# Moving weight loads, their homes and the work behind them: w2a ahead of w2b's third unit, w2b's fifth unit in the loop

## The reference

```
state = gamma*state + k_t v_t^T ;  y_t = q_t state / sqrt(D)          # x = [3072, 512]
logits = x @ phi ; d = softmax over tokens ; slot_input = d.T @ x      # 32 slots, 4 for each of 8 experts
slot_out[e] = relu(slot_input[e] @ w1a[e]) @ w2a[e]                    # w1a [8,512,1024], w2a [8,1024,512]
x2 = softmax over slots(logits) @ slot_out
noisy = x2 @ w_gate + log1p(exp(x2 @ w_noise)) * noise ; top 2 of 8
out[token] += weight * (relu(x2[token] @ w1b[e]) @ w2b[e])             # w1b [8,512,1024], w2b [8,1024,512]
```

## Time and profile before

| | |
|---|---|
| median of 3 runs | 618.42 us (618.32 to 619.48) |
| the profiled execution, its own time | 620.97 us |
| its span, first to last instruction | 619.3 us |
| PE busy | 526.3 us, 85% |
| DVE, ACT, POOL busy | 276.9, 193.1, 250.3 us |
| mean granted TensorE clock | 0.916 of full |
| DMA moved | 107.88 MB, mean 174 GB/s |

### The profile page before, as it was taken

How to read it: one execution, slowest core, us unless ns; L and a number is a source line. 1 busy time by engine, 2 the same in 40 slices (tenths; PEclk the granted TensorE clock), 3 DMA queues, 4 the chain that set the end, 5 groups by cost and what they waited for, 6 DMA issues and landing times.

```text
span 619.3 us, 13374 instructions
## 1 busy us (share of the span) xinstructions
PE 526.3 (85%) x4842; PEld 309.7 (50%) x4843; DVE 276.9 (45%) x427; ACT 193.1 (31%) x357; POOL 250.3 (40%) x218
## 2 busy tenths in 40 slices
PE   4989989796871456575999999999999999999992
PEld 4767667674451343242445545554555445455451
DVE  3536456553654056954578333333323323332330
ACT  0212112121466142464695222222222222222120
POOL 1222122121010000306556766766666666666553
PEclk9989999998795666776999999999999999999997
DMA  6889897886897999958241222212223331433410
GB/s 234 291 278 338 305 335 272 320 299 223 293 380 270 387 399 404 411 237 283 57 151 39 51 44 49 53 35 44 52 43 56 47 47 30 52 44 44 54 18 2
DMA packets 48803, 107.88 MB, mean 174 GB/s; under 512 B 11481, under 2 KB 12745, under 8 KB 48768
## 3 DMA queue, kind: packets, MB, share of 16 engines
q1 hardware_dynamic: 34512, 92.89, 41.6%
q0 software_dynamic: 14256, 14.49, 13.3%
HBM read 93.87 MB, written 29.70 MB: 200 GB/s over the span
## 4 chain that ended last, share of the span: by engine, by line
PE 72%; DMA 14%; DVE 5%; issue 3%; ACT 2%; SPq 0%; POOL 0%; DVEq 0%; ACTq 0%
PE ps L862 45%; DMA w_region<-moe_w 8%; DMA w_region<-chunks 5%; PE ps L845 4%; PE ps L618 3%; PE ps L574 3%; PE ps L721 3%; PE ps L613 3%; PE ps L604 2%; PE ps L625 2%; DVE w_region L1249 1%; PE ps L777 1%; PE ps L648 1%; DMA ident_stack<-consts 1%; PE ps L587 1%
## 5 line engine op out<-in xcount | busy, mean ns | idle before, releaser
L862 PE MATMUL ps<-w_region,s_region 128*128 x1320 | 296.6, 381 | 1.2 <-ACT s_region L1038 1.2
L862 PEld LDWEIGHTS ps<-w_region,s_region 128*128 128x128 f16 x1320 | 127.6, 98 | 146.2 <-issue 5.8
L1432 DVE SCALAR_TENSOR_TENSOR s_region<-ps,s_region 128x1024 f16<-128x1024 f32 x55 | 67.3, 1224 | 184.8 <-ACT s_region L1038 181.9
L1038 ACT ACTIVATE s_region<-ps 128x1024 f16<-128x1024 f32 x55 | 56.3, 1024 | 79.5 <-PE ps L845 50.2
L542 POOL DMA_INDIRECT out<-s_region,rec_region x42 | 71.5, 1702 | 13.5 <-issue 12.5
L536 POOL DMA_INDIRECT out<-s_region,rec_region x42 | 47.4, 1129 | 66.8 <-DVE s_region L1446 66.8
L530 POOL DMA_INDIRECT rec_region<-records,idx x55 | 58.0, 1054 | 18.5 <-issue 18.5
L1028 ACT ACTIVATE s_region<-rec_region 128x128 f16 (+1 forms) x55 | 17.0, 309 | 129.5 <-DMA rec_region<-records,idx 129.5
L744 PE MATMUL ps<-w_region,sw_region 128*32 128x128 f32 x512 | 23.2, 358 | 29.9 <-DMA w_region<-moe_w 29.3
L470 POOL TENSOR_TENSOR s_region<-w_region,s_region 128x512 f32<-128x512 f32 x14 | 14.6, 1044 | 62.5 <-DMA w_region<-chunks 58.5
L1446 DVE TENSOR_SCALAR s_region<-ps,rec_region,y_scale 128x512 f32<-128x512 f32 x42 | 33.9, 806 | 6.4 <-PE ps L862 4.0
(11 more groups left out here) (221 smaller groups left out, 605.5 us busy)
## 6 DMA issues: line engine op xcount, KB each, us to landing
w_region<-moe_w SPq DMA_DIRECT2D x19, 2048.0 KB, 17.0
w_region<-chunks SPq DMA_DIRECT2D x32, 512.0 KB, 6.6
w_region<-moe_w SPq DMA_DIRECT2D x24, 512.0 KB, 7.4
s_region<-moe_w SPq DMA_DIRECT2D x5, 2048.0 KB, 19.1
sw_region<-chunks SPq DMA_DIRECT2D x16, 512.0 KB, 6.3
s_region<-moe_w SPq DMA_DIRECT2D x4, 512.0 KB, 6.9
w_region<-moe_w SPq DMA_DIRECT2D x2, 1024.0 KB, 6.7
out<-s_region,rec_region POOLq DMA_INDIRECT x84
```

The costliest lines, as they stand in the source:

```text
L862: last = nc.tensor.matmul(bank[6 + r], h[:, r, f, :], w2b_parts[:, bass.ds(e, 1), part, f, :].rearrange("p e m -> p (e m)"), start=(first ...
L1038: nc.scalar.activation(h_hi[:, r, :, :].rearrange("p c t -> p (c t)").rearrange("p (a n) -> p a n", a=2), ps[:, 2 + 2 * r:4 + 2 * r, :], A ...
L1432: nc.vector.scalar_tensor_tensor(out=h_lo[:, r, :, :].rearrange("p c t -> p (c t)").rearrange("p (a n) -> p a n", a=2), in0=ps[:, 2 + 2 * ...
```

## The change

Parts of it, with the new line numbers:

- **Loads.** The order is w2b 0, w2b 1, w2a 0 to 7, w2b 2, w1b 0 to 3, w2b 3, w1b 4 to 7, w2b 4 to 7. Every unit has a semaphore of its own, and new homes: w2a in units 4, 5, 6, 8, 2, 3, 4, 5; w1b in 6, 3, 4, 5, 6, 4, 5, 6; w2b arrives in 9, 7, 8, 7, 5, 6, 7, 8. The load of w1b 7 waits for the product with w1b 4. The loads of w2b 6 and 7 wait for the low part of w2b 3.
- **Division.** The slots are no longer divided by their sums before the w1a products; the ReLU's output is multiplied by the inverse instead (one number for each of its rows). The sum over the four row groups is a product with a small matrix `same`, after the first w1a product.
- **PE order.** The c transposes come after the third w2a product. After sort third 0 and the spreads of experts 0 and 1 come w1b 4, sort thirds 1 and 2, the spreads of 2 and 3, w1b 5 to 7.
- **w2b.** Unit 2's sums stand behind softplus, its high half ahead of `sw_sums(0)`; unit 3's sums behind `sw_high(3)`, its high half ahead of `sw_sums(5)`; unit 3's second low half, and all of unit 4 to 7, come in the loop. Units 2 and 3 are summed in two pieces.

```diff
-        w2b_in = [stage_b, w_ring[3], stage_a, stage_b, stage_a, w_ring[2], w_ring[3], stage_a]
+        w1a_home = [unit(u) for u in (4, 5, 6, 0, 8, 1, 2, 3)]
+        w2a_home = [unit(u) for u in (4, 5, 6, 8, 2, 3, 4, 5)]
+        w1b_home = [unit(u) for u in (6, 3, 4, 5, 6, 4, 5, 6)]
+        w2b_in = [unit(u) for u in (9, 7, 8, 7, 5, 6, 7, 8)]
...
 # SyncE: load_w2b(e), load_w2a(e), load_w1b(e)
                 elif e == 2:
-                    sp.wait_ge(ring_used, DC + 1)
-                elif e <= EARLY:
-                    sp.wait_ge(w2b_lo_ready, 1 if e == 3 else 3)
-                elif e < E - 1:
-                    sp.wait_ge(ring_used, 2 * E + e + 2)
+                    sp.wait_ge(ring_used, E + 4)
+                elif e == 3:
+                    sp.wait_ge(w2b_lo_ready, 2)
+                elif e < 6:
+                    sp.wait_ge(ring_used, 2 * E + e + 3)
                 else:
-                    sp.wait_ge(w2b_lo_ready, EARLY + 1)
+                    sp.wait_ge(w2b_lo_ready, 4)
...
+            def load_w2a(e):
+                sp.wait_ge(ring_used, (1, 2, 3, 5, 7, 8, E + 1, E + 2)[e])
...
+            def load_w1b(e):
+                sp.wait_ge(ring_used, (E + 3, E + 6, E + 7, 2 * E, 2 * E + 1, 2 * E + 3, 2 * E + 4, 2 * E + 5)[e])
...
 # ScalarE
-                if e < EARLY:
-                    act.wait_ge(ring_used, DC + e + 1 if e > 0 else DC)
-                elif e < EARLY + 2:
-                    act.wait_ge(ring_used, 2 * E + e + 1)
+                if e <= EARLY:
+                    act.wait_ge(ring_used, (4, 6, E + 5, 2 * E + 2, 2 * E + 6)[e])
                 else:
                     act.wait_ge(w2b_lo_ready, e)
...
+            w2b_sums(4, junk)
             h_high(1, 1)
...
-                if i in (3, 5):
-                    w2b_sums(EARLY + (i + 1) // 2, junk)
-                if i in (4, 6, 8):
-                    w2b_high(EARLY + i // 2 - 1)
+                if i in (4, 6):
+                    w2b_sums(4 + i // 2, junk)
+                if i in (3, 5, 7, 8):
+                    w2b_high({3: 4, 5: 5, 7: 6, 8: 7}[i])
...
 # VectorE
-            join_den()
-            dve.wait_ge(den_spread, 1)
-            link(nc.vector.tensor_scalar(inv_den[:, :], bank[0][:, 0:SL], 1e-9, None, ALU.add))
-            link(nc.vector.reciprocal(inv_den[:, :], inv_den[:, :]))
             dve.wait_ge(slot_in_turned, 1)
...
-            nc.vector.tensor_scalar(h1_4, bank[5][:, 0:F // REP], 0.0, None, ALU.max).then_inc(h1_kept, 1)
+            nc.vector.tensor_scalar(h1_4, bank[5][:, 0:F // REP], 0.0, inv_den[:, 0:1], ALU.max,
+                                    ALU.mult).then_inc(h1_kept, 1)
...
+                if i == 0:
+                    w2b_low(3, (1,))
+                if i in (0, 2, 4, 5):
+                    e = {0: 4, 2: 5, 4: 6, 5: 7}[i]
                     w2b_scale_by_sum(e)
                     scale_y(slice(e, e + 1))
-                if i in (0, 2, 4, 6):
-                    w2b_low(EARLY + i // 2)
+                if i in (1, 3, 5, 6):
+                    w2b_low({1: 4, 3: 5, 5: 6, 6: 7}[i])
```

More of the change, by code:

```diff
@@ L453, in _ @@
             for e in range(E):
-                load_ring(w2a, e, E + e)
-                if e in (2, 5):
-                    load_w2b(2 + e // 5)
+                load_w2a(e)
+            load_w2b(2)
             for e in range(E):
-                load_ring(w1b, e, 2 * E + e)
+                load_w1b(e)
                 if e == 3:
-                    load_w2b(EARLY)
-            for e in range(EARLY + 1, E):
+                    load_w2b(3)
+            for e in range(EARLY, E):
                 load_w2b(e)
@@ L509, in _ @@
             nc.gpsimd.memset(h1_blocks, 0.0).then_inc(blocks_zeroed, 1)
-            for e in range(EARLY):
+            for e in range(3):
                 w2b_all_sum(e)
@@ L724, in _ @@
                 last.then_inc(ring_used, 1)
-            pe.wait_ge(c_ready, 1)
-            for i in range(NT // REP):
-                last = nc.tensor.transpose(bank[2 + i // 4][:, i % 4 * P:(i % 4 + 1) * P],
-                                           c_prob[:, i * REP:(i + 1) * REP, :].rearrange("p t s -> p (t s)"), ident[:, :])
-            last.then_inc(c_turned, 1)
+                if e == 0:
+                    pe.wait_ge(den_ready, 1)
+                    nc.tensor.matmul(bank[0][:, 0:2], same, den[:, :], start=True, stop=True).then_inc(den_spread, 1)
             pe.wait_ge(h1_kept, 1)
@@ L812, in _ @@
                              stop=True).then_inc(ranks_done, 1)
-            for e in range(1, 6):
+            for e in range(1, 4):
                 sw_product(e)
@@ L1009, in _ @@
                 sw_high(e)
+            w2b_sums(3, junk_mid)
+            for unit in range(4):
+                sw_keep(unit)
+            sw_sums(4)
+            act.wait_ge(w2b_sum_ready, w2b_sums_of(4))
+            for unit in range(4, 8):
+                sw_keep(unit)
+            w2b_high(3)
             sw_sums(5)
-            w2b_high(EARLY)
-            for unit in range(8):
-                sw_keep(unit)
             sw_sums(6)
@@ L1280, in _ @@
             w2b_low(0)
-            for e in range(1, EARLY):
-                w2b_scale_by_sum(e)
-                w2b_low(e)
+            w2b_scale_by_sum(1)
+            w2b_low(1)
             dve.wait_ge(iotas_ready, 6)
```

136 lines of the change are left out of this document (67 added, 69 removed).

## The result

The changed kernel takes 614.25 us, median of 20 runs (610.46 to 619.17), against 619.48 us (614.61 to 622.71) for the kernel before in 20 runs on the same chip: ratio 0.9922, interval [0.9897, 0.9947]. The forecast was 608.3, range 603.8 to 613.2. It is faster, as forecast, but by 5.2 us instead of 10.1, and the time lies 1.1 us above the range. The forecast started from 618.42, the median of three runs; with the ratio taken on that start the time would be 613.6, still above the range. Ratios here compare the fast runs of both kernels; a run more than 1.5% above the fastest of its kernel is left out of them.

The account below looks back on a forecast made before the run. DMA supply was taken to bound the stretch ahead of the loop, PE alone the loop. A loop start 14.5 us earlier less 4.4 us of loop stalls gave 10.1 us off 618.42: 608.3 us, range 603.8 to 613.2.

Parts of the forecast that it names:

- w2a's loads: Weight loads ahead of the ranks: w2a 7 lands 17.3 us earlier, from two w2b units (10.5), the hole (5.4), the division (1.3).
- the stretch from the ranks to the loop: From the rank product at 226.8 to the loop start at 277.0, a loop start 14.5 us earlier than before.
- the first stall: In the loop at tile 5's turn, PE waits 2.6 us because w2b 6's load lands late and holds up ACT.
- The hole of 5.4: DMA supply gap between w2a 2 and w2a 7, where SP waits for w2b's low part; removing it gains 5.4 us.
- The division: Slot reduction ahead of w1a starts at once, without the division's chain: 1.3 us gained for w1a and the loads behind.
- Up to the ranks: From the last w2a product's start to the rank product: 18.5 us of DVE, ACT and PE work, unchanged.
- ACT becomes late: Between ranks and group 0's scales, unit 2's high half queues ahead of w1b's first sums on ACT, costing 1.3 us.
- The last w1b unit and the tail: Ahead of the loop: w1b 7 lands at 264.2, group 1's scales come at 264.5, the loop starts 12.5 us later.
- Second stall: In the loop at tile 9's turn, PE waits 1.8 us because unit 6's later low part delays ACT's unit 7 half.
- Rival 2: Products before the loop run at half clock and ACT's queue is longer: 3 to 6.8 us less gain, 611.5 to 615.1; chance 0.20.
- Rivals 1, 3 and 4: No loop stalls, 603.9 (0.14); w2b 6 landing after 24 us, 622.3 (0.05); supply not holding front, no change (0.05).

Follow-up runs that it names:

- e3: Changed kernel with w2b 2 loaded right behind w2a 2 again and w2a 3 waiting in unit 7's buffer: 623.01 us, ratio 1.0052 to the kernel before.
- e1: Changed kernel with the second low half of w2b 3 done ahead of the token loop: 610.88 us, ratio 0.9875 to the kernel before.
- e2: Changed kernel with w2b 3's second low half ahead of the loop and unit 7's high and low halves one tile later: 611.64 us, ratio 0.9872.
- e5: The kernel before, unchanged, run and profiled once more: ratio 1.0008 to the kernel before.
- e4: The kernel before with only the division moved behind w1a's products, into the ReLU: 620.06 us, ratio 0.9997 to the kernel before.
- e7: Changed kernel with the high half of w2b 2 behind the first four w1b sums on ScalarE instead of ahead: 617.21 us, ratio 0.9953 to the kernel before.

## Why the prediction was right and wrong

Where it failed: three terms of the sum were mis-sized (w2a's loads, the stretch from the ranks to the loop, the first stall), and one is missing (the slow products behind that stall).

- **Mechanism and places: right.** e3 shows that the order of the loads carries the front, e1 and e2 that the loop gives back what w2b 6 and the low part of unit 6 make it wait. No gap that wasn't forecast appears in the first nine tiles; what appears is a slow product.
- **w2a's loads: mis-sized, 14.9 us instead of 17.3.** Counted from T the mean goes from 69.7 to 54.8. From w2a 2 to w2a 7 the gain was 14.5 us instead of 16.0. The hole of 5.4 came from one execution with 42.3 us from w2a 2 to w2a 7; e5 and e4 had 40.7 and 40.4. And a unit took 5.40 us (27.00 for five, from the rows above), not 5.27, so that seven of them leave 4.5 us for the hole in the first profile and 3.0 in e5. The division brought 0.4 us up to w2a 2 instead of 1.3. The kernels of the later runs that are the same up to there put it at about 0.8, and the gain at w2a 7 at 15.2.
- **Up to the ranks: 18.5 us, right on average** (19.6, 18.6, 17.0).
- **ACT becomes late: too dear by 1.4.** Group 0's scales came 16.8 behind the ranks, not 18.2; e7 shows why.
- **The last w1b unit and the tail: 1.2 us too cheap, with the 1.4 us above counted in.** Ranks to loop was forecast as 50.2 us; it was 49.6, 52.7 and 52.6, against 47.4 and 47.8 before, so 4.0 more instead of 2.8. Group 0 to group 1 took 20.2 to 21.3 instead of 19.5, since the product with w1b 4 ran mostly at the lower clock where I had counted 2.0. From group 1 to the loop I took the 12.5 of the earlier trace rows; the kernel before had 13.5 in e5 and the changed one 14.7 and 14.4, of which 2 are the late read-out. w1b 7's load took 7.7, 8.1 and 9.2 us from issue to landing instead of 9.9 and left waits of 1.1, 0.9 and 1.9 us.
- **First stall: mis-sized, 3.5 to 3.8 us instead of 2.6** (how much later the turn comes than right behind the work ahead of it). The load was issued at +11.7 from the loop's start, as forecast (+12.05), landed after 11.0 us instead of 9.9, and TensorE had come to the turn 0.4 earlier. The 9.9 of the earlier trace rows was the load of w2b 7 by itself; here w2b 7's load follows 0.4 us behind w2b 6's, which I had not counted. No run has w2b 6 alone, so whether the extra 1.1 us come from that is not shown. The estimate by the Trainium skill ("DMA: Bandwidth & Descriptors", section "Anatomy of one DMA": 6.8 us for this load) is 4.2 us short of the 11.0 measured.
- **What the stall sets off: missing.** 1.7 us at the lower clock behind it in two of three executions. No step of the sum and no rival had it.
- **Second stall: right.** 1.8 us at tile 9 in all three, counted in the same way (TensorE idle for 1.66).
- **Rivals.** Rival 2 (clock and queue, 3 to 6.8 us less gain, to 615.1) comes nearest: the time lies in its span, by other terms in part. Its half clock came true for the product with w1b 4, not for that with w1b 7 (1.9 us in all three). Rivals 1, 3 and 4 are out: the loop stalls, w2b 6 lands in 11 and not 24 us, and the front follows w2a 7.

The sum as it came out: front 10.9 (14.9 at w2a 7, 4.0 given back up to the loop), loop -6.5, together 4.4 of forecast 10.1. 3.6 of the missing 5.7 are the front's (2.4 w2a's loads, 1.2 the stretch from the ranks to the loop), 2.1 the loop's (1.1 the first stall, about 1.1 the slow products, as a mean of the three).

## What to carry to other kernels

A gap read from one execution is a sample: count every stretch from an event behind which the program is the same, and take two executions before a term is sized from it. A wait of TensorE in a dense stretch can cost more than its length: here nothing was added behind waits of up to 3.1 us, and 1.7 us behind four of five waits of 3.4 us and more. Before a duration is taken from a load that was alone, ask which load is issued right behind it in the new order. When an early phase is pulled forward, ask of each later load whether its buffer is freed by work that didn't move.
